# Fourteen attention steps ahead of the MLP: normalisation and reciprocals moved forward in their queues, the values' preparation spread over two more half steps

## The reference, cut to what matters

```python
# attention: q, k, v are (4, 8, 768, 64); n_sink 4, window 128
scores = scale * np.matmul(q, k.transpose(0, 1, 3, 2))
scores = np.where(keep, scores, -1e9)            # keep: sink keys, or the last 128
a = np.exp(scores - scores.max(-1, keepdims=True))
a = a / (a.sum(-1, keepdims=True) + 1e-09)
x = np.matmul(a, v)                              # -> 3072 tokens x 512
# MLP
h = x @ w_in                                     # 512 x 2048
x = (h - np.tanh(h)) @ w_out                     # 2048 x 512
# experts
logits = x @ w_gate + modality_bias[modality_id]
e_idx = np.argmax(logits, axis=1)                # one of 8, weight from the softmax
out[mask] = gate_w[mask, None] * (np.maximum(x[mask] @ w1[e], 0.0) @ w2[e])
```

## Time and profile before

| | us |
|---|---|
| median of 3 runs | 1076.66 |
| lowest and highest | 1076.42, 1077.22 |
| the profiled execution | 1072.89 |
| span of its core in the trace | 1071.3 |
| busy in the span: PE, DVE, ACT, POOL | 993.2, 649.5, 581.6, 327.6 |

### The profile page before, as it was taken

One profiled execution on the slowest core, in us unless ns is written; L12 is line 12 of the kernel. 1 busy time (PEld: TensorE's weight loads), 2 busy tenths in 40 slices (PEclk: granted clock), 3 DMA queues, 4 the chain that ended last, 5 costly groups with the idle time before them and its releaser, 6 DMA issues.

```text
span 1071.3 us, 23847 instructions
## 1 busy us (share of the span) xinstructions
PE 993.2 (93%) x7968; PEld 607.1 (57%) x7968; DVE 649.5 (61%) x2272; ACT 581.6 (54%) x1329; POOL 327.6 (31%) x462
## 2 busy tenths in 40 slices
PE   1757998999999999999999999999899999899996
PEld 0524444555554565555455555555487777677773
DVE  5665767667767767777866775646765334633331
ACT  3767777666657765766666675536422224522221
POOL 4776675112116211213511210101122322232322
PEclk9858999999999999999999999999999999999998
DMA  8710001201100220100110010041025111111111
GB/s 308 262 35 19 18 19 65 78 19 36 48 18 19 63 80 19 49 18 19 37 48 19 22 45 1 2 166 51 1 51 183 68 54 47 40 40 49 49 49 38
DMA packets 24375, 60.30 MB, mean 56 GB/s; under 512 B 9504, under 2 KB 9760, under 8 KB 22752
## 3 DMA queue, kind: packets, MB, share of 16 engines
q1 hardware_dynamic: 15392, 45.77, 12.7%
q0 software_dynamic: 5728, 13.43, 4.0%
q10 hardware_dynamic: 3168, 0.02, 0.2%
HBM read 45.35 MB, written 14.12 MB: 56 GB/s over the span
## 4 chain that ended last, share of the span: by engine, by line
PE 74%; DVE 11%; ACT 6%; issue 5%; POOL 2%; DVEq 1%; DMA 0%; ACTq 0%; SPq 0%; POOLq 0%
PE h_ps L751 18%; PE acc L807 18%; PE s_ps L1856 6%; PE h_ps L1907 6%; PE pt_ps L1856 6%; PE acc L1907 5%; PE pt_ps L639 3%; PE s_ps L569 3%; PE x_out L706 2%; ACT probs L587 1%; PE s_ps L858 1%; DVE pt_lo L648 1%; DVE qk_top L401 1%; PE pt_ps L662 1%; PE x_out L1833 1%
## 5 line engine op out<-in xcount | busy, mean ns | idle before, releaser
L807 PE MATMUL acc<-w_out_all,g_hi 128*128 128x512 f16 x768 | 228.4, 379 | 0.0
L751 PE MATMUL h_ps<-xt_hi,w_in_all 128*128 128x384 f16 x960 | 196.4, 327 | 4.6 <-DVE g_raw L772 3.0
L807 PE MATMUL acc<-w_out_all,g_lo 128*128 128x512 f16 x384 | 146.0, 380 | 3.3 <-DVE g_lo L792 2.7
L751 PEld LDWEIGHTS h_ps<-xt_hi,w_in_all 128*128 128x128 f16 x960 | 91.2, 100 | 62.3 <-issue 7.0
L807 PEld LDWEIGHTS acc<-w_out_all,g_hi 128*128 128x128 f16 x768 | 75.1, 98 | 77.7
L763 ACT ACTIVATE g_raw<-h_ps,batch_scale 128x384 f32<-128x384 f32 x120 | 69.7, 581 | 88.5 <-PE h_ps L751 84.5
L792 DVE SCALAR_TENSOR_TENSOR g_lo<-g_raw,batch_scale,g_hi 128x384 f16<-128x384 f32 x128 | 84.7, 662 | 44.5 <-ACT g_hi L782 44.5
L782 ACT ACTIVATE g_hi<-g_raw,batch_scale 128x384 f16<-128x384 f32 x128 | 77.9, 608 | 55.3 <-DVE g_raw L772 53.8
L101 POOL TENSOR_TENSOR tick<-tick 1x1 f32<-1x1 f32 x83 | 15.5, 187 | 295.4 <-ACT y L1923 117.5
L751 PE MATMUL h_ps<-xt_lo,w_in_all 128*128 128x384 f16 x480 | 98.3, 328 | 0.0
L580 DVE CUSTOM_DVE_ANT_0 probs<-s_ps,mask 128x260 f32<-128x260 f32 (+1 forms) x192 | 70.2, 402 | 45.5 <-issue 38.1
(11 more groups left out here) (315 smaller groups left out, 2104.9 us busy)
## 6 DMA issues: line engine op xcount, KB each, us to landing
qk_raw<-in_qk SPq DMA_DIRECT2D x31, 454.0 KB, 3.4
raw<-in_w SPq DMA_DIRECT2D x16, 512.0 KB, 8.5
v_raw<-in_v SPq DMA_DIRECT2D x4, 1536.0 KB, 7.9
x_tokens<-x SPq DMA_DIRECT2D x24, 256.0 KB, 2.5
w_in_all<-in_w_in SPq DMA_DIRECT2D x4, 1024.0 KB, 9.6
w_out_all<-in_w_out SPq DMA_DIRECT2D x4, 1024.0 KB, 9.9
x_tokens<-g_raw SPq DMA_DIRECT2D x1, 1024.0 KB, 12.4
vs_raw<-in_v SPq DMA_DIRECT2D x24, 4.0 KB
```

What stands on the lines that cost most here:

```text
L751: mm = eng.matmul(h_of(m, f), w16[0][:, f, x * DM + k * P:x * DM + (k + 1) * P], r[:, par, k, :], start=(i == 0), stop=(i == 3 * KD - 1))
L807: mm = eng.matmul(acc[t][:, :], l[f % 2][:, t * P:(t + 1) * P], w16[1][:, f, x * DM:(x + 1) * DM], start=(f == 0 and i == 0), stop=(f == N ...
```

## The change

Three things change, all inside `alone`, that is for pairs 0 to 13.

1. On ACT, `normalise(r)` stood at the end of the first half step, behind `split_x`, `prepare_alone`, `conversions` and `transpose_sinks`. It now stands directly behind the high half of the transposes of r - 1 (L644).
2. On DVE, `normalise(r)` (the reciprocals) stood behind `gather_sinks(r - 1)` and the low half of the transposes of r - 1. It now stands ahead of both. The mask of r + 1 follows as before.
3. The values of batch 0: the six maxima go two each to the half steps 0, 2 and 3 (before: three each to 0 and 2). `spread`, `v_scales` and the first three `v_multiply` go from half step 2 to 3. The splits of blocks 0, 1, 2 go from the half steps 2, 3, 4 to half step 4, all three.

```diff
         def prepare_alone(E, eng, i):
 
-            if i in (0, 2):
-                for blk in range(TPC):
-                    v_tops(E, eng, 0, TPC * (i // 2) + blk)
-            if i == 2:
+            if i in (0, 2, 3):
+                v_tops(E, eng, 0, (0, 2, 3).index(i) * 2)
+                v_tops(E, eng, 0, (0, 2, 3).index(i) * 2 + 1)
+            if i == 3:
                 if E in ("dve", "pe"):
                     spread(E, eng, 0)
                 v_scales(E, eng, 0)
                 for blk in range(TPC):
                     v_multiply(E, eng, 0, blk)
-            if i in (2, 3, 4):
-                v_split(E, eng, 0, i - 2)
             if i == 4:
+                for blk in range(TPC):
+                    v_split(E, eng, 0, blk)
                 sink_multiply(E, eng, 0)
@@
                 if E == "act":
                     score_pair(E, eng, r)
                     stage(transpose_probs, E, eng, r - 1)
+                    normalise(E, eng, r)
                     stage(split_x, E, eng, r - 2)
                 if E == "dve":
+                    normalise(E, eng, r)
                     stage(gather_sinks, E, eng, r - 1)
                     stage(transpose_probs, E, eng, r - 1)
-                    normalise(E, eng, r)
                     if r + 1 < ALONE:
                         score_pair(E, eng, r + 1)
                     stage(split_x, E, eng, r - 2)
@@
                 if E == "act":
                     stage(transpose_sinks, E, eng, r - 1)
-                    normalise(E, eng, r)
                 prepare_alone(E, eng, 2 * r + 1)
                 conversions(E, eng, 2 * r + 1)
```

## The result

| | before | after |
|---|---|---|
| median of 20 runs each, same chips | 1075.09 us | 1072.53 us |
| lowest and highest | 1072.02, 1077.22 | 1069.71, 1074.47 |
| ratio, 95% interval | | 0.9977, 0.9968 to 0.9985 |
| profiled execution | 1072.89 us | 1070.08 us |
| its span | 1071.3 us | 1068.1 us |

The change makes the kernel 0.23% faster, some 2.5 us, and the interval allows 1.6 to 3.4. A second measurement beside the experiments gave 0.9972 (0.9960 to 0.9984).

The account below looks back on a forecast made before the run. From the MLP on PE's products bound the kernel (93% busy), so only their start at 86.07 us could move: 0.9 + 1.5 + 0.7 - 0.2 = 2.9 us earlier, 1076.66 - 2.9 = 1073.8 us, range 1071.0 to 1077.4.

Parts of the forecast that it names:

- The values' scale stays at 21.8: At the end of DVE's queue: the scale stays at 21.8 us, the moved maxima cost or bring nothing.
- Term 1: Start of exp(3): 0.9 us earlier, as the queries' low half moves into POOL's earlier pause; bounds 0 and 3.1.
- Term 2: From exp(3) to exp(4): 1.5 us gained by normed(3) running right behind pt_hi(2), ahead of the transposed sinks.
- Term 3: Steps 4 to 8: ACT hardly waits for reciprocals, 0.7 us gained in steps 4 and 5 together; bounds 0 and 2.6.
- POOL carries the 3.1 us on: From step 6: POOL's weight splits set the pace and pass on the keys' 3.1 us lead, adding nothing.
- rival B: Steps 5, 9, 12: ACT waiting at normed(r) becomes the bound, 1079.4 us; chance 0.12, of which 0.08 slower.
- Term 4: Steps 9 to 13, where scale chains make DVE late: a price of 0.2 us, first MLP product at 83.2.
- The gather beside POOL: Where ACT waits for DVE's gather: by the shared-port page, long again (723 ns, not 209) whenever POOL is busy.
- The shift passes through the MLP: MLP stage: its queues wait for other engines, not a fixed time, so the 2.9 us shift should pass.
- rival C: TensorE's clock at the MLP's start: 1075.2 or 1072.0 us; chances shared with other rivals, 0.28 bad side, 0.10 good side.

Follow-up runs that it names:

- splits_late: Kernel before with only the first three value splits moved to half step 4; in its trace the first MLP product came at 84.40 us.
- order_alone: Kernel before with only parts 1 and 2 (normalise early on ACT, reciprocals first on DVE), values as before; ratio 0.9994 (0.9982 to 1.0005).
- values_alone: Kernel before with only part 3 (the values' preparation), normalise in its old place on both engines; ratio 0.9986 (0.9974 to 0.9998).
- act_old_order: Changed kernel with ACT's normalise back in its old place (parts 2 and 3 remain); first MLP product at 84.67 us.
- four_old: Changed kernel with normalise in its old place on both engines for pairs 6, 9, 12 and 13; ratio to the kernel before 0.999 (0.9979 to 1.0001).
- after_again: The changed kernel measured and traced once more, no edit; ratio to the kernel before 0.9972 (0.9960 to 0.9984).
- old_dve_order: Changed kernel with DVE's reciprocals back behind the gather and pt_lo (parts 1 and 3 remain); ratio to the kernel before 0.9998 (0.9986 to 1.001).
- sinks_later: Changed kernel with the sink values' multiplication and halves two half steps later (6 and 7); ratio to the kernel before 0.9985 (0.9973 to 0.9996).
- splits_late_timed: The same kernel as splits_late, timed and traced again; ratio to the kernel before 0.9988 (0.9975 to 1.0001).

## Why the prediction was right, and where not

**The time.** I forecast 2.9 us and 1073.8; the medians differ by 2.6 us. My number stands 1.3 us above the measured 1072.53 because the kernel before lies 1.6 us lower in its 20 runs (1075.09) than in the 3 from which I started (1076.66). But the first MLP product moved by 1.83 us (1.95 counted from exp(0)) and not by 2.9. The median is nearer to my number than the mechanism was, and that nearness is luck: at equal clock the fit leaves 1.7 us of the 2.6, and what the clock of these runs added was in no term of mine. The interval of the ratio, 1.6 to 3.4 us, holds both.

**The values' scale stays at 21.8.** Right: 21.98 for POOL's start against 21.93, with a trace that starts 0.12 us later.

**Term 1, 0.9 us at exp(3).** Right: 0.95 counted from exp(0), through POOL's pause as described. But it was not what mattered: splits_late has none of it and the same end within the spread of the traces.

**Term 2, 1.5 us in step 3.** The size was right (5.96 to 4.37 us, so 1.59) and the cause mostly wrong. I gave it to the early place of normed(3). order_alone leaves exp(4) where it was, and splits_late gets 1.27 us with no reordering. The cause is the keys' lead, which lets PE finish its weight sums before exp(3). I had noted that those start earlier, and had not seen that the transposes stood behind them. The order adds 0.7 us to it (values_alone takes 5.06 us for this step).

**Term 3, 0.7 us in steps 4 and 5.** From exp(4) to exp(6) it was 0.34 us (9.25 to 8.91). Step 6 added 0.27 us, though the gather there took 1.06 us; at exp(7) the lead was 3.15 us from exp(0), close to the 3.1 that I carried.

**"POOL carries the 3.1 us on."** Wrong: exp(7) to exp(9) took 8.35 us before and 8.99 after, so 0.64 us were lost. The keys' low half of load 3 started 2.37 us earlier (57.41 to 55.04), not 3.1. In step 7 ACT's weight split now stands behind normed(7) and comes at 50.36, and POOL, whose queue had no such pause there, waits 0.48 us for it. act_old_order and values_alone, which leave ACT's normed(7) in its old place, take 8.3 us from exp(7) to exp(9) as before, so it is ACT's move that costs here. That is rival B in small: what waits behind normed(r) is POOL's feed. four_old, which takes normed(9) out of the way, makes step 10 0.6 us shorter.

**Term 4, -0.2 us.** Too small: from exp(9) to the MLP it took 26.76 us before and 27.32 after, so 0.56 us. ACT stood 2.99 us at normed(9), with the gather as last releaser, and pt_lo(11), which stands behind the reciprocals now, started 1.32 us earlier only (78.82 to 77.50), so the sinks and the transposes of pair 12 came at 80.44 and not at 79.4. I had the mechanism and the place, and worked with a lead that POOL had already cut: the scale chain let the reciprocals of pair 9 start at 61.77, and I had put them near 61.0. The sum is 0.95 + 1.59 + 0.34 + 0.27 - 0.64 - 0.56 = 1.95.

**The gather beside POOL.** Right as a mechanism: 1.06 us from 43.94, while POOL subtracts from 43.79 to 44.94. It is not long whenever POOL is busy, as I had put it: in the kernel before it took 0.21 us from 46.27, though POOL multiplied from 46.22 to 46.93. The Trainium skill's rule of the shared port pair (page "SBUF — State Buffer", section "Who interferes with whom") agrees with the first: the copy ended when POOL's subtraction had, at 45.00 for 44.94. In step 3 I allowed for 0.5 us and it was 0.28.

**The shift passes through the MLP.** Right but for the clock, my rival C. In the trace of the changed kernel the first twelve products took 4.03 us and not 3.58, and the next ones came only 1.39 us earlier (91.22 to 89.83). In after_again another 1.5 us went, with the same program. So the group in which a trace falls is not decided by the kernel alone.

**A term that nobody had.** In every run on record with its span, for every kernel with DVE's reciprocals moved forward (part 2), 1.9 to 2.0 us of the time lie outside the span; for the kernel before, values_alone, splits_late and old_dve_order it is 1.5 to 1.6. So part 2 costs some 0.4 us of device time that no view of the span shows: of the 1.95 us at the MLP some 1.6 are left, close to the 1.7 of the fit. The cause is open.

**What stays open.** Why more of the change's runs had the higher clock than runs of the kernel before, and whether the earlier work does that. With the clock taken out, of the change's three parts the traces and the fit give all of the gain to the move of the three value splits, though its ratio alone, 0.9988 with an interval from 0.9975 to 1.0001, does not show a gain. values_alone lies even 0.7 us below the change there, of which the 0.4 us outside the span are a part. A difference of 1 us between two kernels is at the limit of these runs.

## What to carry to other kernels

An instruction that waits at the head of a queue costs what stands behind it, and on other engines what that feeds: here three value splits held back the keys' conversion on POOL, through it 32 weight sums on PE, and through them the transposes. Moving them was worth as much at the MLP as the whole change, within the 0.3 us by which two traces of one kernel differ. When an instruction is moved forward in one queue, its inputs must move forward on the engine that makes them, or the move costs (3.2 us here); and what it pushes back should be read as somebody's feed. A lead at the start of a chain of engines is worth little until it is followed to the last instruction of the stretch: 3.15 us at exp(7) were 1.95 us at the first MLP product, and the 3.6 us of sinks_later were nothing one step on. And a difference of 2 us in 1070 is to be read at equal granted clock, which is recorded with each run; else the clock's draw is taken for the kernel's.

## What the runs showed of the hardware

TensorE's granted clock rose from 1.2 to 2.4 GHz at different moments in two executions of one program with nearly the same work before it: by 90 us in one, after 92 us in the other, at a price of some 1.5 us. Over all 14 traces the way from the first MLP product to the instruction near 777 us took 691.1 to 691.5 us in the nine in which the clock was back in the stretch from 90 to 92 us (mean 0.89 or more), and 692.7 to 693.4 in the five in which it was not (0.56 or less). splits_late and splits_late_timed, again one kernel, fall in different groups too. The Trainium skill, page "TensorE: Matmul & The Clock Gate", Part 1, says that activity releases the throttle; the traces agree, and show that nearly the same activity does not release it at the same time.

A second difference of 1.6 to 2.9 us lies behind 777 us: 292.4 us to the end in the trace of the changed kernel and 292.5 in act_old_order, and 294.1 to 295.3 in the others. The clock goes with this one too. In these two traces it stays at 1.00 while PE makes its last products (1056 to 1060 us); in the twelve others it falls to 1.2 GHz for a while there (mean 0.80 in the kernel before, 0.81 in values_alone, 0.88 in after_again). PE's pause ahead of these products is the same 2.36 us in all 14 traces. So 1.7 of the 3.2 us by which the span of the first trace was shorter lie behind 777 us, go with the clock there, and are not what the change moved.
